# Attention, a cosine MLP and a routed mixture of experts: rows listed by expert in DRAM, block by block

## The reference

```python
# 1. attention in windows: 4 x 8 heads, 768 queries, chunks of 32; keys: 8 memory + 16 left + 32 + 8 right
a = softmax(scale * q_c @ k_full.T);  x = a @ v_full            # -> [3072, 512]
# 2. dense layer, d_ff = 2048
h = x @ w_in;  x = (h * cos(h)) @ w_out
# 3. routed experts: E = 8, F = 1024, one expert a row, and only for some rows
do_compute = x @ w_skip > 0
e_idx = argmax(x @ w_gate);  gate = softmax(x @ w_gate)[e_idx]
out = x
out[do_compute] = x + gate * (relu(x @ w1[e_idx]) @ w2[e_idx])
```

## Time and profile before

| | |
|---|---|
| median of three runs | 922.83 us |
| the profiled execution | 920.39 us, span 918.7 us |
| PE busy | 841.1 us (92%) |
| PEld (weight load) busy | 745.2 us (81%) |
| DVE busy | 525.8 us (57%) |
| ACT busy | 468.6 us (51%) |
| POOL busy | 49.4 us (5%) |
| DMA | 97.38 MB, mean 106 GB/s |

### The profile page before, as it was taken

One profiled execution on the slowest core, in us unless ns is written; L12 is line 12 of the kernel. 1 busy time (PEld: TensorE's weight loads), 2 busy tenths in 40 slices (PEclk: granted clock), 3 DMA queues, 4 the chain that ended last, 5 costly groups with the idle time before them and its releaser, 6 DMA issues.

```text
span 918.7 us, 20139 instructions
## 1 busy us (share of the span) xinstructions
PE 841.1 (92%) x7922; PEld 745.2 (81%) x7923; DVE 525.8 (57%) x1030; ACT 468.6 (51%) x809; POOL 49.4 (5%) x57
## 2 busy tenths in 40 slices
PE   4799999999999999999999999999994688999995
PEld 3788878887987887788878878888983587999994
DVE  3577655545556455455545564554457576666664
ACT  2566655555556455555555564554443255444442
POOL 0000000000000000000000000000011211111110
PEclk9999999999999999999999999999997799999998
DMA  9811131112113110311121122002016355665653
GB/s 345 286 59 41 42 106 57 59 59 93 59 59 100 63 59 26 104 59 59 56 95 59 56 96 69 24 1 70 1 36 217 115 215 212 227 214 217 221 195 113
DMA packets 40685, 97.38 MB, mean 106 GB/s; under 512 B 5852, under 2 KB 5852, under 8 KB 40608
## 3 DMA queue, kind: packets, MB, share of 16 engines
q1 hardware_dynamic: 37632, 90.21, 28.6%
q0 software_dynamic: 2976, 6.05, 1.8%
HBM read 82.34 MB, written 16.79 MB: 108 GB/s over the span
## 4 chain that ended last, share of the span: by engine, by line
PE 77%; DVE 7%; ACT 7%; issue 4%; DMA 3%; POOL 1%; SPq 0%; ACTq 0%; POOLq 0%; DVEq 0%
PE h_ps L686 26%; PE y_ps L700 24%; PE h_ps L787 8%; PE y_ps L802 7%; PE s_ps L642 5%; ACT L839 2%; DMA xg<-x_mid,idx_from 2%; PE s_ps L606 2%; PE turn L621 1%; ACT L890 1%; PE turn L654 1%; ACT us L867 1%; PE y_ps L642 1%; DMA k_pre<-qk 1%; PE turn L664 1%
## 5 line engine op out<-in xcount | busy, mean ns | idle before, releaser
L686 PE MATMUL h_ps<-xT_hi,in_hi 128*128 128x384 f32 x512 | 179.2, 350 | 2.6 <-DVE xT_lo L1023 1.4
L686 PE MATMUL h_ps<-xT_hi,in_lo 128*128 128x384 f32 x512 | 172.8, 337 | 0.0
L686 PE MATMUL h_ps<-xT_lo,in_hi 128*128 128x384 f32 x512 | 172.4, 337 | 0.0
L866 ACT ACTIVATE hs<-h_ps 128x384 f32<-128x384 f32 x128 | 62.7, 490 | 199.8 <-PE h_ps L686 199.8
L700 PE MATMUL y_ps<-out_hi,g_hi 128*128 128x512 f32 x384 | 151.9, 396 | 4.8 <-DVE g_lo L1100 4.8
L700 PE MATMUL y_ps<-out_hi,g_lo 128*128 128x512 f32 x384 | 151.8, 395 | 0.0
L700 PE MATMUL y_ps<-out_lo,g_hi 128*128 128x512 f32 x384 | 151.3, 394 | 0.0
L1094 DVE TENSOR_SCALAR whole<-us 128x384 f32<-128x384 f32 x128 | 47.2, 368 | 124.2 <-ACT us L867 124.2
L686 PEld LDWEIGHTS h_ps<-xT_hi,in_hi 128*128 128x128 f32 x512 | 96.7, 189 | 8.3 <-issue 1.6
L890 ACT ACTIVATE us<-us 128x384 f32<-128x384 f32 x128 | 67.2, 525 | 68.8 <-DVE us L1096 68.5
L686 PEld LDWEIGHTS h_ps<-xT_lo,in_hi 128*128 128x128 f32 x512 | 96.8, 189 | 2.5
(11 more groups left out here) (147 smaller groups left out, 1243.7 us busy)
## 6 DMA issues: line engine op xcount, KB each, us to landing
raw<-w SPq DMA_DIRECT2D x72, 512.0 KB, 5.4
k_sb<-qk SPq DMA_DIRECT2D x22, 512.0 KB, 4.6
v_sb<-v SPq DMA_DIRECT2D x22, 512.0 KB, 3.5
x_mid<-x SPq DMA_DIRECT2D x24, 256.0 KB, 3.7
out<-x SPq DMA_DIRECT2D x24, 256.0 KB, 3.7
q_sb<-qk SPq DMA_DIRECT2D x22, 256.0 KB, 2.7
in_raw<-w_in SPq DMA_DIRECT2D x4, 1024.0 KB, 14.7
out_raw<-w_out SPq DMA_DIRECT2D x4, 1024.0 KB, 15.2
```

Of the source, the lines that this page charges most:

```text
L686: last = pe.matmul(h_ps[:, f % 2, 0:BN], w[:, dc, f * P:(f + 1) * P], x[:, half, dc, :], start=(n == 0), stop=(n == 3 * DC - 1))
L866: act.activation(hs[:, f % 2, :], h_ps[:, f % 2, 0:BN], ACT.Copy)
```

## The change

1. `chosen` is kept for one block only. Each block's routing gains three steps: `ranks` (nine matmuls of 8 columns, into `turn`), `place` (five DVE operations, which turn ranks into positions in a list for each expert, and carry `filled_to` on), and a DVE operation `nowhere` that puts skipped rows out of bounds. The third `x1`, `logits`, and `route`, `rexp`, `gate` move to earlier sites.
2. POOL scatters, in each block, pairs (row number, gate) of 8 bytes into `lists` in DRAM, one region of 3072 pairs for each expert; at the start it fills the lists with numbers out of bounds. The gate column of `x_mid` goes.
3. The sort is gone. The first eight slots are the experts in order, without a table; a table for further slots is worked out by DVE behind `rows_low(0)`.
4. POOL loads the slot's 256 pairs (`load_list`) before it gathers; `load_list(s+1)` waits until the scatters of slot s-1 have landed, because they read the same buffer `listed`.
5. `raw1` and `raw2` get two buffers each; SP may load slot s+1 when the low parts of slot s-1 are written.

```diff
-ROUTER = [(4, "x1", 0), (5, "logits", 0), (7, "x1", 1), (8, "logits", 1), (24, "x1", 2),
-          (25, "logits", 2), (26, "route", 0), (27, "rexp", 0), (28, "gate", 0)]
+ROUTER = [(4, "x1", 0), (5, "logits", 0), (7, "x1", 1), (8, "logits", 1), (10, "x1", 2), (11, "logits", 2),
+          (12, "route", 0), (13, "rexp", 0), (14, "gate", 0), (17, "ranks", 0), (18, "place", 0)]
...
-        raw1 = sb("raw1", [P, DC, EF], offset=O_IN_HI)
-        raw2 = sb("raw2", [P, EFT, D], offset=O_IN_HI + DC * EF * 4)
+        raw1 = [sb("raw1_a", [P, DC, EF], offset=O_IN_HI), sb("raw1_b", [P, DC, EF], offset=O_RING)]
+        raw2 = [sb("raw2_a", [P, EFT, D], offset=O_IN_HI + DC * EF * 4), sb("raw2_b", [P, EFT, D], offset=O_QKV)]
...
+            run(0, 0)
+            with eng.Fori(0, E // 2 - 1) as r:
+                run(2 * r + 1, 1)
+                run(2 * r + 2, 0)
             eng.wait_ge(table_done, 1)
-            used = eng.value_load(table[0:1, NSLOT + 2:NSLOT + 3], min_val=1, max_val=NSLOT)
-            run(0, 0)
-            with eng.Fori(0, NSLOT // 2) as r:
-                with eng.If(2 * r + 1 < used):
-                    run(2 * r + 1, 1)
-                with eng.If(2 * r + 2 < used):
-                    run(2 * r + 2, 0)
+            used = eng.value_load(slots_used[0:1, 0:1], min_val=E, max_val=NSLOT)
+            with eng.Fori(E // 2, NSLOT // 2 + 1) as r:
+                with eng.If(2 * r - 1 < used):
+                    run(2 * r - 1, 1)
+                with eng.If(2 * r < used):
+                    run(2 * r, 0)
...
-            def load_raw(s, expert):
-                wait(sp, w1lo_done, 4 * s)
+            def load_raw(s, par, expert):
+                wait(sp, w1lo_done, 4 * (s - 1))
...
-                wait(sp, w2lo_done, 4 * s)
+                wait(sp, w2lo_done, 4 * (s - 1))
...
+            def sort(R):
+                for j in range(BT):
+                    wait(pool, pairs_st[j], 16 * R)
+                carry(pool)
+                pool.tensor_copy(pairs[:, :, 0:1].bitcast(I32), token[:, :].unsqueeze(2)).then_inc(token_done, 1)
...
+                pool.wait_ge(route_step, ROUTE * (R + 1))
+                carry(pool)
+                for j in range(BT):
+                    pool.indirect_dma_start(
+                        out=lists[:, :], out_offset=bass.IndirectOffsetOnAxis(ap=place[:, j:j + 1], axis=0),
+                        in_=pairs[:, j, :], in_offset=None,
+                        bounds_check=E * N - 1, oob_is_err=False).then_inc(pairs_st[j], 16)
...
+            def load_list(s, par, first):
+                for a in range(2):
+                    wait(pool, scattered[a], 16 * (s - 1))
+                if not isinstance(s, int):
+                    carry(pool)
+                pool.dma_start(listed[:, par, :, :], lists[bass.ds(first, SLOT), :].rearrange("(a p) c -> p a c", p=P)
+                               ).then_inc(list_ld[par], 16)
             def gather(s, par):
-                pool.wait_ge(idx_done, s + 1)
+                pool.wait_ge(list_ld[par], 8 * (s - par + 2))
+                wait(pool, o_done, 2 * (s - 1))
...
             def run_slot(s, par):
+                first = pool.value_load(begins[0:1, bass.ds(s + 1, 1)], min_val=0, max_val=E * N - SLOT)
+                load_list(s + 1, 1 - par, first)
                 gather(s + 1, 1 - par)
...
+            def ranks():
+                for t in range(BT):
+                    for before in range(t):
+                        pe.matmul(turn[:, 0, t * E:(t + 1) * E], ones[:, :], chosen[:, before, :],
+                                  start=(before == 0), stop=False)
+                    pe.matmul(turn[:, 0, t * E:(t + 1) * E], preceding[:, :], chosen[:, t, :], start=(t == 0), stop=True)
+                for t in range(BT):
+                    last = pe.matmul(turn[:, 0, BT * E:(BT + 1) * E], ones[:, :], chosen[:, t, :],
+                                     start=(t == 0), stop=(t == BT - 1))
+                return last
...
+                    if step == "place":
...
+                        then(dve.tensor_tensor(place_e[:, :, :], turn[:, 0, 0:BT * E].rearrange("p (t e) -> p t e", e=E),
+                                               filled_to[:, :].unsqueeze(1).to_broadcast(bc), ALU.add))
+                        then(dve.tensor_tensor(place_e[:, :, :], place_e[:, :, :], chosen[:, :, :], ALU.mult))
+                        then(dve.tensor_reduce(place_f[:, :], place_e[:, :, :], AX.X, ALU.add))
+                        then(dve.tensor_tensor(place[:, :], place_f[:, :], nowhere[:, :], ALU.add))
+                        then(dve.tensor_tensor(filled_to[:, :], filled_to[:, :], turn[:, 0, BT * E:(BT + 1) * E], ALU.add))
...
-                    dve.scalar_tensor_tensor(o_sb[:, a, :], y_ps[:, a, :], xg[:, par, a, D:D + 1], xg[:, par, a, 0:D],
+                    dve.scalar_tensor_tensor(o_sb[:, a, :], y_ps[:, a, :], listed[:, par, a, 1:2], xg[:, par, a, :],
                                              ALU.mult, ALU.add).then_inc(o_done, 1)
```

More of the change, by code:

```diff
@@ L51 @@
 SPLIT_FIRST = 3
-T_STEPS = ("probs", "x1", "logits")
+T_STEPS = ("probs", "x1", "logits", "ranks")
 def steps_of(attention, router):
@@ L188, in program @@
         at[0] = O_XT
[L189 to L204, removed]
-        tiles = sb("tiles", [P, E])
[L206 to L215, removed]
+        xg = sb("xg", [P, 2, 2, D])
+        listed = sb("listed", [P, 2, 2, PAIR])
+        x1T_last = sb("x1T_last", [P, BT, DC * P])
+        iota_slot = sb("iota_slot", [P, MORE])
+        count = sb("count", [P, E])
+        tiles = sb("tiles", [P, E])
+        more_end = sb("more_end", [P, E])
+        more_first = sb("more_first", [P, E])
+        shift = sb("shift", [P, E])
+        from_e = sb("from_e", [P, E])
+        left_e = sb("left_e", [P, E])
+        begun = sb("begun", [P, MORE, E])
+        ended = sb("ended", [P, MORE, E])
+        picked = sb("picked", [P, MORE, E])
+        expert_f = sb("expert_f", [P, MORE])
+        from_f = sb("from_f", [P, MORE])
+        rows_f = sb("rows_f", [P, E + MORE])
+        rows_i = sb("rows_i", [P, E + MORE], I32)
+        experts = sb("experts", [P, E + MORE], I32)
+        begins = sb("begins", [P, E + MORE], I32)
+        slots_used = sb("slots_used", [P, 1], I32)
+        assert at[0] <= O_RING, at[0]
         def ps(name, n):
@@ L513, in _ @@
                       allow_small_or_imprecise_dtypes=True).then_inc(ready, 1)
[L515 to L524, removed]
@@ new lines, in _ @@
+            sort(0)
+            with pool.Fori(1, BLOCKS - 1) as R:
+                sort(R)
+            pool.wait_ge(h_full, BLOCKS * FT)
+            pool.iota(iota_slot[:, :], pattern=[[1, MORE]], base=0, channel_multiplier=0,
+                      allow_small_or_imprecise_dtypes=True)
+            pool.iota(experts[:, 0:E], pattern=[[1, E]], base=0, channel_multiplier=0)
+            pool.iota(begins[:, 0:E], pattern=[[N, E]], base=0, channel_multiplier=0).then_inc(ready, 1)
+            pool.memset(xg[:, :, :, :].rearrange("p s a d -> p (s a d)"), 0.0).then_inc(ready, 1)
@@ L575, in _ @@
             used = slots(pool, run_slot)
+            for n in range(2):
+                pool.wait_ge(xg_ld[n], 32)
+            carry(pool)
             for a in range(2):
@@ L748, in _ @@
             last_logits(2)
-            pe.wait_ge(ready, 5)
-            pe.wait_ge(route_step, ROUTE * BLOCKS - 3)
-            every = chosen[:, :, :].rearrange("p t e -> p (t e)")
-            pe.matmul(s_ps[:, 0, 0:NT * E], before[:, :], every, start=True, stop=True)
-            pe.matmul(s_ps[:, 1, 0:NT * E], ones[:, :], every, start=True, stop=True).then_inc(ranks_full, 1)
-            pe.wait_ge(tile_hot_done, 1)
-            for T in range(NT):
-                if T % LOOK == 0:
-                    pe.wait_ge(sort_step, SORTED + T // LOOK + 1)
-                last = pe.matmul(y_ps[:, 2, 0:3 * NCOL], lo_hot[:, T, :],
-                                 hi_hot[:, T, :, :].rearrange("p a n -> p (a n)"), start=(T == 0), stop=(T == NT - 1))
-            last.then_inc(lookup_full, 1)
+            pe.wait_ge(route_step, ROUTE * (BLOCKS - 1) + CHOSEN)
+            ranks().then_inc(last_ranks_full, 1)
             def turn_rows(s, par):
-                pe.wait_ge(gathered[par], 16 * (s + 2 - par))
+                pe.wait_ge(xg_ld[par], 16 * (s + 2 - par))
                 for a, bank in enumerate((turn[:, 0, :], s_ps[:, 0, :])):
+                    if a == 0 and isinstance(s, int) and s == 0:
+                        pe.wait_ge(route_step, ROUTE * BLOCKS)
                     for dc in range(DC):
@@ L810, in run_slot @@
                     carry(pe)
-                with pe.If(behind < N):
+                with pe.If(rows >= P + 1):
                     second(1)
-                with pe.If(behind >= N):
+                with pe.If(rows < P + 1):
                     pe.wait_ge(ey_full, 2 * s + 1)
@@ L928, in _, with w1_high @@
```

(10 more changed lines are left out.)

289 lines of the change are left out of this document (154 added, 135 removed).

## The result

The changed kernel took 963.59 us (median of 4 runs, 959.14 to 964.18), the kernel before 921.96 us beside it (4 runs, 920.44 to 925.05). The ratio is 1.0437, 95% interval 1.0394 to 1.0479. The forecast was 980 within 940 to 1018; the measured difference is 41.6 us where 57 were forecast. The profiled execution of after took 963.27 us with a span of 961.7, against 920.39 and 918.7 before.

A forecast was written before the change was run, and what follows sets the result against it. The prediction took TensorE to bound the blocks and full slots, with a dip at the passage between. Its terms 21 + 18 + 4.7 + 1 + 12 = 57 on 922.8 gave 980 us, range 940 to 1018 for 8 in 10.

The forecast's parts named there:

- The order of GpSimd in a slot: Expert slots: scatter landing and list load come before the next gather, where the margin was for one DMA trip.
- the likeliest case: Whole kernel: the forecast itself, 980 us, own range 955 to 1005, chance 0.50.
- half way: Rival: scatter at 3.6, list 2.9 everywhere, the rest as forecast, clock kept in full slots; about 945 us, chance 0.13.
- Part 1: Full slots 3 to 7: gathered rows 4.3 us late in each of five, 21 us in all.
- Part 2: Slots 1 and 2: trips of 5.7, 4.8 and 5.7 make rows 9.1 us later in each, together 18 us.
- Part 3: Passage from last block to slot 0: sort removed, ranks, placing and three trips added; 4.7 us later.
- Part 4: The blocks: rank matmuls +4, logits stands -6, crowding at sites 12 and 13 +0.5 in six blocks; together +1 us.
- Crowding: Blocks: rival "crowded blocks", sites 11 to 14 hold TensorE 3 us in six blocks beside the forecast; 995 us, chance 0.10.
- the forecast's own sign of being wrong: Blocks: the forecast is wrong if TensorE stands at sites 12 to 16.
- Part 5: TensorE's clock after stands: 2.7 us per return; 5.4 for slots 1 and 2, 6.8 for full slots, sum 12 us.
- the quiet rival: Whole kernel: each trip lands as its shortest neighbour, 2.4, 2.4, 3.0, no clock loss; 926 us, chance 0.07.
- half each: Full slots: stands of 4.3 us lie at the clock's edge, so half the 2.7 us return is charged each, 6.8 us.

The follow-up runs named there:

- the kernel before with one trip added: Against the kernel before: only a wait added, the gather holds until the scatters of the slot before have landed; 936.65 us, ratio 1.0134.
- the late fill alone: Against the changed kernel: the lists' fill in DRAM is held until four h tiles are done; 960.3 us, ratio 1.0407 to the kernel before.
- the sites alone: Against the kernel before: only the third x1, logits, and route, rexp, gate move to sites 10 to 14; 915.6 us, ratio 0.9924.
- both trips out: Against the changed kernel: lists of all further experts fetched once behind slot 0's gather, row numbers copied out by DVE; 925.66 us, ratio 1.0022.
- one trip out: Against the changed kernel: scatter's row numbers copied out of listed, so the list load needn't wait for the scatter's landing; 944.37 us, ratio 1.0213.

## Why the prediction came out as it did

**The mechanism held.** The order of GpSimd in a slot, told as deciding the case, did: transposes wait for DMA in seven slots, GpSimd's queue stands for the scatter ahead of the list load, and taking out the two trips takes out 38 of 42 us. The direction, and the likeliest case, were right; the total was 15 us too high. Of the signs it named, the waits in seven slots and for the scatter showed; the sizes mostly didn't (4 to 5 us in slots 3 to 7, 10 to 13 in slots 1 and 2, slot 0's `h` at 728 to 730; measured 0.7 to 5.1, 10.6 and 7.3, 727.34). One sum in it is wrong: its "half way" rival, scatter at 3.6 and list at 2.9 everywhere, comes by its own terms to 3.2 late in five slots (16), 5.1 in two (10), 0.6 at the passage, 1 in the blocks and 5.4 of clock, 33 in all and 956 us, not 945. So the measured 963.59 lies nearer to that rival than to the forecast of 980, and its two prices are near those measured in the full slots (3.6 and 2.2). The sizes by part:

| part | forecast | measured |
|---|---|---|
| 1: stands, slots 3 to 7 | 4.3 each, 21 | 2.0, 3.2, 1.2, 5.1, 0.7: 12 |
| 2: slots 1 and 2 | 18 | 10.6 + 7.3 less 2.9: 15 |
| 3: passage to slot 0 | 4.7 | 3.5 |
| 4: end of the last block | +1 | +0.1 |
| 5: clock | 12 | 5.4 + 3.9 + 2.6: 12 |
| other waits and `h` in slots 0 to 2 | not in the sum | -2.3 |
| end of the kernel | not in the sum | 2.7 |

**Part 1 was the term mis-sized.** The list was priced at 2.9, the gate store's median. Once the weights' burst is over it took 2.17 to 2.21 in slots 3 to 6 and 2.52 in slot 7. And the scatter, taken at 4.65 as "half in traffic", is not half anything: it goes with how far the burst has got. SP issues the w1 weights of a later slot at these times:
```profile
862.23 1.91 SPq L494 DMA_DIRECT2D raw_b<-w  x4
...
892.89 1.91 SPq L494 DMA_DIRECT2D raw_a<-w  x4
```
and the chain has the scatters of the same two slots as
```profile
870.30 2.70 DMA out<-o_sb,listed
...
895.13 5.99 DMA out<-o_sb,listed
```
8.1 us behind the issue the scatter lands in 2.70, 2.2 us behind it in 5.99, and in slot 2 2.8 us behind it (779.47 to 782.29) in 6.34. At 5.6 us behind (835.36 to 840.94) it took 4.27, at 6.8 behind (807.10 to 813.86) 2.78, and 2.3 where no burst came. In the kernel before with one trip added it is the same with single buffers: 5.87 at 2.4 us behind (823.33 to 825.72), 3.9 at 5.1 (796.71 to 801.83). The forecast had the weights start "about 3 us sooner" than 814.95, which is 4.5 ahead of its scatter at 816.49, in every slot. For that distance 4.65 is a fair price (with the late fill alone 4.36 at 4.2: 779.80 to 783.99); but the distance was 2.2 to 8.1 from slot to slot, and slot 7 had no burst. The mean of the five in slots 3 to 7 is 3.6, and of their lists 2.25: 1.05 + 0.65 less in each of five slots is 8.5 of the 9 us by which part 1 missed (21 against 12). The hand-over from scatter to list, 0.75 where 1.1 was taken, is most of the rest.

**Part 2** took 5.7, 4.8 and 5.7 for the three trips in both slots. Measured in slot 1: scatter 2.1, list 6.2, gather 6.4; in slot 2: 6.3, 2.2, 4.8. POOL's timeline for slot 1, and SP's queue:
```profile
753.23 1.00 POOL L617 DMA_INDIRECT out<-o_sb,listed  x1 [0.30 <-issue]
756.08 0.76 POOL L586 DMA_DIRECT2D listed<-lists  x1 [1.85 <-DMA out<-o_sb,listed]
763.30 1.05 POOL L595 DMA_INDIRECT xg<-x_mid,listed  x1 [6.46 <-issue]
```
```profile
754.86 1.90 SPq L494 DMA_DIRECT2D raw_b<-w  x4
```
The scatter was issued ahead of the weights and landed in 2.1, the list behind them in 6.2. The gate store's 6.7 beside weights was the right neighbour for a list in a burst, and of the fourteen scatters and lists in the slots four took over 4 us. The sums, 14.7 and 13.3 against 16.2, are nearer than most of their terms: the burst strikes one or two of three, whichever lie in it.

**Part 3** came out near in the sum: the third pair scatter at 706.32 (forecast 705.2), then 6.3 to the list load (with the hand-over), 3.9 to the first gather, 6.1 from the last gather to the transposes. The forecast had 6.8, 5.9 and 5.7 for these three: the list took 2.8 where 4.8 was priced. The table stood behind `h` as forecast; its 23 operations took 5.7 us (4.6 forecast) and TensorE didn't stand for them. What the forecast said and didn't weigh is that the weights' burst, "no longer held by the table", made these trips long: holding it back took 8.8 us off the stand. The forecast priced the burst inside the trips and never by itself.

**Part 4.** The stands at `logits` went (-6, as forecast). The nine rank matmuls of a block start and end within about 0.4 us (499.09 to 499.47 in one), where 0.6 was taken. Crowding is there, but small. PE's waits in the blocks, after, then the kernel with the sites alone:
```profile
PE y_ps L767 <- DVE g_lo L1176: 3.7, 9, 1.4
```
```profile
PE y_ps L700 <- DVE g_lo L1100: 2.2, 2, 1.8
```
VectorE is late with `g_lo`. The first and the last of these stands are in both (0.4 each, then 1.4 and 1.8); the seven between them, 1.9 us, are new. Six are of 0.2 us and lie just ahead of site 17, one in each of six blocks, which is, very small, the forecast's own sign of being wrong ("TensorE stands in the blocks at sites 12 to 16"). In the four blocks timed above five of the seven lie, 1.5 us or 0.4 a block; with the ranks' 0.4 that is the 0.74 that come back. The four blocks are 0.9 us shorter than before, yet the last block's logits end 0.14 us later in after, since the place from which I counted comes 1.7 us later (211.48 against 209.77). In the four kernels whose start and blocks are those of after that end lies between 695.7 and 698.3, so I don't lay the 1.7 to the fill.

**Part 5.** The clock's loss was 12, as forecast, but by luck. Five of the seven restarts were cold, where the forecast had two and five halves, and one cost 2.1 (1.1 in the transposes, 1.0 in `y`) where 2.7 was taken; what made up for it is 1.3 more in slot 0's `h`, which the forecast had left as it was.

**The Trainium skill beside the runs.** The page "DMA: Bandwidth & Descriptors", section "Anatomy of one DMA — SWDGE (gpsimd) path", gives 2.0 us fixed plus the bytes at 436 GB/s, by which a list would take 2.0 and a scatter of 128 rows 2.6 (estimates from its figures). Without a burst the trace is near it (2.2 to 2.5, and 2.1 to 2.8). Beside a burst it isn't (5.8 to 6.2 for the 2 KB list, 6.0 to 6.3 for the scatter), and the packet by packet turns of "Queues, rings and completion order" don't lead one to expect that either. Trips all of that size are near the quiet rival, 926; the measured 963.59 lies between it and the forecast.

**What stays open.** The end of the kernel: 11.7 us from the last scatter to the end, 9.0 before. It is 9.9 in the kernels with both trips out (916.65 to 926.5) and 11.7 with one out (930.14 to 941.8), so it goes with something of the code behind the slots; no engine is busy in most of it. And the half of the 2.3 us above that no wait accounts for.

## What to carry to other kernels

Before moving data that one step needs next from SBUF to DRAM, count the DMA trips in series between the last producer and the consumer, and what slack the consumer has: here a slot had room for one trip, each further one cost 14 to 19 us over seven slots. A buffer from which an indirect DMA reads its row numbers is kept here until that DMA has landed; copying the few index columns out with a DVE instruction, or fetching all lists once, takes that wait out of the series. And a weight prefetch started at the first possible moment can lengthen the small trips that the critical path is made of: let it wait until they have landed.

## What the hardware showed that was not expected

**Small transfers beside a burst.** A 2 KB list load took 2.2 us by itself and 6.2 beside a 2 MB burst of weights on another queue. The second scatter of a slot, which ends last, took 2.3 by itself and 6.0 to 6.3 beside a burst. It is named for 128 rows, 256 KB, but moves only those rows of the slot that lie behind the 128th. What GpSimd's queue moved from 925.60 to 928.20, and from 895.10 to 901.20 (packets, MB, share of 16 engines):
```profile
q0 software_dynamic: 80, 0.03, 4.3%
```
```profile
q0 software_dynamic: 80, 0.12, 5.3%
```
So the scatter of 2.34 us moved 0.03 MB and that of 5.99 moved 0.12, and that of 6.34, issued in slot 2 for slot 1's rows, had none to move, since slot 1 has no row behind the 128th. The prediction priced it by a full 256 KB. The price went with the burst's phase; how much size adds no pair of rows here isolates.

**The clock behind a stand isn't told by the stand's length.** TensorE's timeline, first the kernel with one trip out, then the changed kernel with the late fill; a transpose group of 1.11 is at the lower level, one of 0.65 at the higher:
```profile
838.34 1.11 PE L829 MATMUL turn<-ident,xg 128*128 128x128 f32 x4 [3.20 <-DMA xg<-x_mid,listed]
...
891.28 0.65 PE L829 MATMUL turn<-ident,xg 128*128 128x128 f32 x4 [3.24 <-DMA xg<-x_mid,listed]
```
```profile
797.17 0.66 PE L830 MATMUL turn<-ident,xg 128*128 128x128 f32 x4 [4.08 <-DMA xg<-x_mid,listed]
```
Stands of 3.20 and 3.24 us end differently, one of 4.08 ends at full clock, and in after one of 1.98 ended cold (stretch; length, busy PE, PEld, DVE, ACT, POOL, granted clock, DMA share, GB/s):
```profile
825.50:828.00 2.50, 2.46 (x10) 2.37 (x11) 1.58 (x2) 1.06 (x2) 0.00 (x0) 0.50 0.33 26
```
0.50 is 1.2 GHz. What decides between them no run here isolates; costing "half each" for stands near 2 to 4 us was as good as these rows allow.
